# A fused attention, soft mixture and feed-forward kernel: the recurrence's transposes made whole, and the logits computed slot by slot

## The chip, the cores and the metric

One core of a Trainium2 chip runs the kernel. The metric is the device time of one execution in microseconds (us). Everything is float32, or float32 split into two rounded parts.

## What is computed

The input is r, k, v of shape (4 batches, 8 heads, 768 tokens, 48), a decay w and a bonus u per head. The reference runs three stages, one after the other:

```python
for t in range(S):                       # a linear-attention recurrence, per batch and head
    cur = einsum('bhd,bhe->bhde', u * k_t, v_t)
    y_t = einsum('bhd,bhde->bhe', r_t, state + cur)
    state = w * state + einsum('bhd,bhe->bhde', k_t, v_t)
x = y, as (3072 tokens, 384)
logits = x @ phi                         # soft mixture: 32 slots, 8 experts of 4 slots
disp = softmax(logits over tokens);  slot_in = disp.T @ x
slot_out = per expert: relu(slot_in @ w1) @ w2
x = softmax(logits over slots) @ slot_out
out = (relu(x @ w_in) ** 2) @ w_out      # feed-forward, 384 -> 2048 -> 384
```

## The kernel before

**Units.** The recurrence is cut into 6 chunks of 128 tokens and, inside a chunk, into 4 pairs of heads (hp = 0 to 3). A chunk and a pair make a unit, n = 4c + hp, 24 in all; a unit holds all 4 batches, and a chunk is worked in two halves of 64 tokens. The two heads of a pair lie at partitions 0 to 47 and 64 to 111 (HEAD_ROWS), so that TensorE's array is used as four 64x64 tiles: most products are 16 small matmuls, and the profile counts two MATMUL records for each (x32). In one unit TensorE does, in this order, own_step of the unit before (scores times values, L949), on hp = 1 only the logits of the chunk before (logit_parts, L880), scores_step (L911), keys_step (the next unit's keys transposed, turn_keys, L899), carried_step (queries times the old state, L934), state_step (keys times values, L922), carried_rest (L934), and turn_step (the output of the unit before transposed to tokens on partitions, turn_x, L890).

**Transposes and logits.** turn_keys and turn_x are ordinary matmuls against a piece of the identity, 16 of 64x64 or 48x48 each. logit_parts is 64 matmuls per chunk (x128 records) of 48 rows by 32 slots, the two heads of a pair kept apart in two halves of the PSUM tile turn_ps, which VectorE then adds (add_logits, L730). turn_ps has two banks and serves four uses in turn: the logits, the transposed keys, the transposed x, and the powers of the decay before the loop. So keys_step(n) waits for keep_x of the earlier unit (x_done), turn_step waits for keep_keys (k_done), and after the logits keys_step waits for VectorE's sum (lg_free).

**The other engines.** ScalarE does per unit keep_x (L532, two copies into x_sb), copy_y (L519, PSUM to x_t), keep_keys (L508) and scale_bonus (L501). VectorE does mask_scores (L701, L705), advance (L716, L720) and scale (L691). GpSimd does keep_state (L449) and turned_keys (L431), which weights the natural-order keys of a unit three ahead. SyncE issues the loads in a written order: per unit keys_in, two recept, values and one 512 KB piece of w1. Semaphores alone order the engines.

**Code.** The block of TensorE writes the chunk loop as a hardware loop, `with pe.Fori(0, CH) as c:` (L1033), whose body holds the four units of a chunk; all other engines have their 24 units written out. Later, groups 1 to 4 of the feed-forward stage are a hardware loop on TensorE, ScalarE and VectorE (L1220), with a body of 208 matmuls.

**Before the loop.** GpSimd makes the identity, masks (const_step), clears recept buffers, values of unit 3 and state_a (L424, the last of it after the load values_in[1]), makes fold4 (L438), then weights keys 0 to 2. VectorE computes powers of w; TensorE turns them (L1020) and VectorE copies them to kn_pow (L674). ScalarE clears PSUM and x_t (L538 to L544). Then keys_step and state_step of unit 0 run and the loop begins (L1033).

**After the loop.** own_step of unit 23, the logits of the last chunk (three pairs ahead of y_copied, the last pair behind it), turn_x into score_ps, the column maxima, gather (L1066, disp.T @ x), the experts (L1114, L1139), the mix, and the feed-forward stage (L1176, L1198), which runs from about 210 us to the end.

Of the kernel before, what the change touches and what calls it, by code (L numbers as in the profile page):

```python
# [12 lines left out]
P = 128  # L13
# [48 lines left out]
def program(nc, rk_t, rkv_n, w_t, u, phi, w1, w2, w_in, w_out, out):  # L62
# [35 lines left out]
    keys_n = [place(f"keys_n{i}", [P, B, 2, D]) for i in range(HP)]  # L98
# [5 lines left out]
    state_next = place("state_next", [P, HP, B, D])  # L104
# [3 lines left out]
    disp = place("disp", [P, TILES, SLOTS])  # L108
    x_t = place("x_t", [P, HP, B, P])
    q_pow = place("q_pow", [P, HP, SUB])  # L110
    state_b = place("state_b", [P, HP, B, D])
# [65 lines left out]
    with stack:  # L177
# [5 lines left out]
        with phase:  # L183
# [5 lines left out]
            turn_ps = bank("turn_ps", 2 * BANK)  # L189
# [18 lines left out]
        back_cleared = sem("back_cleared")  # L208
        ps_cleared = sem("ps_cleared")
# [25 lines left out]
        x_done = sem("x_done")  # L235
        logit_mm = sem("logit_mm")
# [62 lines left out]
        def _(sp):  # L299
# [4 lines left out]
            def load_params():  # L304
                by_head = u.rearrange("(a h d) -> h d a", h=2, d=D)
# [89 lines left out]
        def _(pool):  # L395
# [23 lines left out]
            pool.wait_ge(back_cleared, R_BUFS - 2)  # L419
            nc.gpsimd.memset(values[HP - 1][:, :, :], 0.0).then_inc(carried_done, 1)  # L420
            for hp in range(HP):
                if hp == HP - 1:
                    pool.wait_ge(values_in[1], 16)
                nc.gpsimd.memset(state_a[:, hp], 0.0).then_inc(state_a_ready, 1)  # L424

            def turned_keys(n):
# [4 lines left out]
                nc.gpsimd.tensor_tensor(keys_n[n % HP][:, :, :, :],  # L431
# [3 lines left out]

            for q in range(QUADS):
                rows = slice(SLOTS * q, SLOTS * (q + 1))
                chained(nc.gpsimd.tensor_copy(fold4[rows, :].rearrange("p (a s) -> p a s", s=SLOTS),  # L438
                                              ident[rows, rows].unsqueeze(1).broadcast_to([SLOTS, QUADS, SLOTS])))
# [15 lines left out]
            pool.wait_ge(kn_pow_done, 1)  # L455
            for n in range(HP - 1):
                turned_keys(n)
# [38 lines left out]
        def _(sc):  # L496
# [7 lines left out]
            def keep_keys(n):  # L504
# [3 lines left out]
                nc.scalar.activation(  # L508
                    keys[n % 2][0:PAIR].rearrange("p b (s t) -> p s b t", t=SUB),
                    turn_ps[0:PAIR, :].rearrange("p (s b t) -> p s b t", s=2, t=SUB)[:, :, 0:B], ACT.Copy,  # L510
                    scale=w_64_inv[0:PAIR, n % HP:n % HP + 1]).then_inc(k_done, 1)

            def copy_y(n):
# [4 lines left out]
                wait(sc, logit_mm, c + 1)  # L518
# [31 lines left out]
            for n in range(UNITS):  # L550
                if n >= 2:
                    keep_x(n - 2, turn_ps)
# [713 lines left out]
```

## Time and profile before

| | us |
|---|---|
| median of 3 runs | 448.79 |
| lowest, highest | 444.84, 472.27 |
| the profiled execution | 445.05 |
| its span, first to last instruction | 443.3 |

The profiled execution is one run, 3.74 us under the median; its span is 1.75 us shorter than its time. Times in rows are counted from the start of the span. Busy time of an engine says nothing by itself; what counts is which work or wait stands in the chain that ends last. PE is TensorE's matmuls, PEld its weight loads, DVE VectorE, ACT ScalarE, POOL GpSimd, SP SyncE, PEclk the clock granted to TensorE as a share of 2.4 GHz.

### The profile page before, as it was taken

The numbers are of one execution on the slowest core, as the hardware profiler recorded it, in microseconds if no ns is written. First come the engines' busy times: TensorE is split into PE (matmuls) and PEld (weight loads), VectorE is DVE, ScalarE is ACT, GpSimd is POOL, SyncE is SP. The second block draws the span as 40 slices with busy tenths as digits, with TensorE's granted clock in tenths as the row PEclk, the third lists the DMA queues.
The fourth block names the chain that finished last, engine by engine and source line by source line (L and its number), as shares of the span: only waits on it lengthen the run. The fifth ranks groups of instructions, "written<-read, shape, count | busy, mean of one in ns | idle before, by whom it ended". The sixth has DMA issues, their size and how long they took to land.

```text
span 443.3 us, 16892 instructions
## 1 busy us (share of the span) xinstructions
PE 390.5 (88%) x7284; PEld 354.4 (80%) x7284; DVE 245.6 (55%) x395; ACT 199.2 (45%) x351; POOL 56.0 (13%) x91
## 2 busy tenths in 40 slices
PE   0767799479699987996699999999999999999997
PEld 0666799478599842353699999999999999999996
DVE  6324387325366637115966655565665566566553
ACT  4214365323255511126345654565465455546542
POOL 4421124211232001105600000000000000000000
PEclk9968899866699968999699999999999999999999
DMA  5536478562469299995000020010010001001001
GB/s 142 166 104 206 151 243 242 174 204 88 138 227 310 63 368 371 375 404 185 1 0 1 1 72 1 1 71 0 0 70 1 0 0 71 0 0 71 0 1 71
DMA packets 29027, 50.93 MB, mean 115 GB/s; under 512 B 3777, under 2 KB 23233, under 8 KB 28609
## 3 DMA queue, kind: packets, MB, share of 16 engines
q1 hardware_dynamic: 28992, 50.44, 34.0%
q8 instruction: 26, 0.43, 0.4%
q14 instruction: 9, 0.07, 0.1%
HBM read 45.71 MB, written 4.72 MB: 114 GB/s over the span
## 4 chain that ended last, share of the span: by engine, by line
PE 86%; issue 7%; DVE 3%; SPq 1%; ACT 1%; DMA 1%; POOL 1%; DVEq 0%; POOLq 0%; ACTq 0%
PE out_ps L1198 46%; PE score_ps L911 7%; PE h_ps L1176 5%; PE turn_ps L890 4%; PE turn_ps L880 4%; PE turn_ps L899 3%; PE y_ps L934 3%; PE y_ps L949 3%; PE wide L1114 3%; PE inc_ps L922 3%; PE wide L1139 2%; PE wide L1066 1%; DVE act_lo L857 1%; ACT x_sb L532 1%; PE wide L1125 1%
## 5 line engine op out<-in xcount | busy, mean ns | idle before, releaser
L1198 PE MATMUL out_ps<-w_hi,act_hi 128*128 128x384 f32 x384 | 130.9, 341 | 5.1 <-DVE act_lo L857 5.1
L1198 PE MATMUL out_ps<-w_hi,act_lo 128*128 128x384 f32 x384 | 131.3, 342 | 0.0
L1198 PE MATMUL out_ps<-w_lo,act_hi 128*128 128x384 f32 x384 | 131.0, 341 | 0.0
L852 DVE TENSOR_TENSOR act<-relu_h 128x512 f32<-128x512 f32 x96 | 68.8, 716 | 78.7 <-ACT relu_h L620 78.7
L620 ACT ACTIVATE relu_h<-h_ps 128x512 f32<-128x512 f32 x96 | 57.3, 597 | 101.2 <-PE h_ps L1176 100.3
L1198 PEld LDWEIGHTS out_ps<-w_hi,act_hi 128*128 128x128 f32 x384 | 72.9, 190 | 6.2 <-ACT act_hi L623 3.8
L1198 PEld LDWEIGHTS out_ps<-w_lo,act_hi 128*128 128x128 f32 x384 | 73.2, 191 | 3.8
L1198 PEld LDWEIGHTS out_ps<-w_hi,act_lo 128*128 128x128 f32 x384 | 72.8, 190 | 0.0
L857 DVE TENSOR_TENSOR act_lo<-act,act_hi 128x512 fp32r<-128x512 f32 x96 | 68.4, 712 | 4.6 <-ACT act_hi L623 1.0
L623 ACT ACTIVATE act_hi<-relu_h 128x512 fp32r<-128x512 f32 x96 | 60.8, 634 | 3.9
L701 DVE TENSOR_TENSOR scores<-score_ps,ident_sub 128x512 f32<-128x512 f32 x24 | 16.6, 692 | 47.9 <-PE score_ps L911 47.9
L911 PE MATMUL score_ps<-queries,keys 48*64 48x128 f32 x768 | 35.0, 318 | 8.3 <-issue 8.3
L1176 PE MATMUL h_ps<-mix_t,gin 128*128 (+1 forms) x96 | 37.9, 396 | 0.4 <-DVE gin L834 0.4
L508 ACT ACTIVATE keys<-turn_ps,w_inv 112x512 f32<-112x512 f32 x24 | 16.5, 687 | 43.9 <-PE turn_ps L899 43.9
L911 PEld LDWEIGHTS score_ps<-queries,keys 48*64 48x64 f32 x768 | 28.0, 161 | 9.6 <-issue 9.6
L519 ACT ACTIVATE x_t<-y_ps 112x512 f32<-112x512 f32 x25 | 14.9, 597 | 29.5 <-PE turn_ps L880 20.2
L431 POOL TENSOR_TENSOR keys_n<-keys_in,kn_pow 128x384 f32<-128x384 f32 x24 | 24.6, 1028 | 28.2 <-DMA keys_in<-in_rkv_n 28.0
L899 PE MATMUL turn_ps<-ident_sub,keys_n 64*48 64x64 f32 x800 | 21.3, 247 | 7.3 <-POOL keys_n L431 7.3
L899 PEld LDWEIGHTS turn_ps<-ident_sub,keys_n 64*48 64x48 f32 x800 | 20.2, 146 | 7.5 <-issue 7.4
L949 PE MATMUL y_ps<-scores,values 64*48 64x64 f32 x800 | 19.3, 239 | 6.4 <-issue 6.1
L934 PE MATMUL y_ps<-queries,state_a 48*48 48x64 f32 x384 | 23.0, 233 | 0.0
L890 PE MATMUL turn_ps<-ident,x_t 48*64 48x48 f32 x768 | 19.1, 231 | 4.3 <-issue 4.2
(149 smaller groups left out, 436.9 us busy)
## 6 DMA issues: line engine op xcount, KB each, us to landing
w_sb<-in_w SPq DMA_DIRECT2D x21, 512.0 KB, 4.4
w_room<-in_w SPq DMA_DIRECT2D x4, 1536.0 KB, 13.5
keys_in<-in_rkv_n SPq DMA_DIRECT2D x24, 192.0 KB, 4.2
recept<-in_rk_t SPq DMA_DIRECT2D x48, 96.0 KB, 3.6
values<-in_rkv_n SPq DMA_DIRECT2D x24, 192.0 KB, 2.6
out_dram<-y_sb SPq DMA_DIRECT2D x5, 768.0 KB, 3.6
w_x<-in_w SPq DMA_DIRECT2D x2, 1536.0 KB, 13.4
w_w<-in_w SPq DMA_DIRECT2D x4, 768.0 KB, 10.0
```

The costliest lines, as they stand in the source:

```text
L431: nc.gpsimd.tensor_tensor(keys_n[n % HP][:, :, :, :], keys_in[n % K_BUFS][:, :, :].rearrange("p b (h d) -> p b h d", h=2), kn_pow[:, hp].u ...
L620: nc.scalar.activation(relu_h[f % 2][:, :], h_ps[f % 4][:, :], ACT.Relu).then_inc(relu_done, 1)
L623: nc.scalar.activation(act_hi[f % 4][:, :], relu_h[f % 2][:, :], ACT.Square).then_inc(act_hi_done, 1)
L852: nc.vector.tensor_tensor(act[f % 2][:, :], relu_h[f % 2][:, :], relu_h[f % 2][:, :], ALU.mult).then_inc(act_done, 1)
L857: nc.vector.tensor_tensor(act_lo[f % 4][:, :], act[f % 2][:, :], act_hi[f % 4][:, :].bitcast(F32), ALU.subtract).then_inc(act_lo_done, 1)
L890: last = nc.tensor.matmul(bank[HALVES[s], at:at + D], x_t[HEAD_ROWS[r], hp, b, HALVES[s]], ident[HEAD_ROWS[r], HEAD_ROWS[r]], start=True, ...
L899: last = nc.tensor.matmul(turn_ps[HEAD_ROWS[h], at:at + SUB], keys_n[i][HALVES[s], b, h], ident_sub[HALVES[s], :], start=True, stop=True)
L911: last = nc.tensor.matmul(score_ps[part, at:at + P], keys[hp % 2][rows, b, part], queries[hp][rows, b, s].rearrange("p k t -> p (k t)"), s ...
L934: return nc.tensor.matmul(y_ps[head_rows(b, h), at:at + SUB], state[HEAD_ROWS[h], hp, b], queries[hp][HEAD_ROWS[h], b, s, 0], start=(s == ...
L949: return nc.tensor.matmul(y_ps[head_rows(b, h), at:at + SUB], values[hp][HALVES[s], b, D * h:D * (h + 1)], scores[hp % 2][HALVES[s], h, b] ...
L1176: nc.tensor.matmul(h_ps[f % 4][:, :], gin[:, P * f:P * (f + 1)], mix_t[:, bass.ds(g * B, B), :], start=True, stop=True).then_inc(h_mm, 1)
L1198: last = nc.tensor.matmul(out_ps[t][:, 0:DM], a[f % 4][:, tok], w[:, f], start=(f == 0 and i == 0), stop=(f == NF - 1 and i == 2))
```

## The change

- turn_keys and turn_x become 4 whole transposes each (128x128, and 112 rows in). turn_ps is split into two banks: x_ps for x and the logits, kt_ps for the keys. For that keys_n gets 64 columns a head in place of 48, with the 16 extra cleared (GpSimd), and phi_sb is cleared before its load (VectorE; SyncE waits for it, phi_cleared).
- The logits are computed transposed: pair_logits is 8 matmuls, stationary phi (112x32), moving x_t (112x256), each pair in its own 32 columns of the array, so that each pair's 32 slots are rows of x_ps. ScalarE copies that to the new logits_t (keep_logits_t); token_logits, 4 matmuls with logits_t stationary and 32 columns of fold4 moving, adds the four pairs and turns the result to tokens; ScalarE copies it to logits (keep_logits). VectorE's add_logits goes.
- On hp = 1, keys_step moves ahead of the logits, keep_keys ahead of copy_y, and token_logits stands between state_step and carried_rest.
- Before the loop, TensorE gets two runs of 7 matmuls of the identity with itself (keep_awake), into score_ps. The powers are turned into x_ps and kt_ps, with no PSUM clear ahead of them; VectorE copies them in two. GpSimd weights the keys of unit 0 right after kn_pow, ahead of fold4 and of the last piece of state_a.
- After the loop, pair_logits of the last chunk stands whole behind y_copied.
- state_next and state_b change places in memory; state_b now lies on disp, which is written only after the loop.

```diff
-    keys_n = [place(f"keys_n{i}", [P, B, 2, D]) for i in range(HP)]
+    keys_n = [place(f"keys_n{i}", [P, B, 2, SECOND]) for i in range(HP)]
...
-            turn_ps = bank("turn_ps", 2 * BANK)
+            x_ps = bank("x_ps")
+            kt_ps = bank("kt_ps")
...
             pool.wait_ge(back_cleared, R_BUFS - 2)
+            for i in range(HP):
+                nc.gpsimd.memset(keys_n[i][:, :, :, D:], 0.0)
             nc.gpsimd.memset(values[HP - 1][:, :, :], 0.0).then_inc(carried_done, 1)
-            for hp in range(HP):
-                if hp == HP - 1:
-                    pool.wait_ge(values_in[1], 16)
+            for hp in range(HP - 1):
                 nc.gpsimd.memset(state_a[:, hp], 0.0).then_inc(state_a_ready, 1)
...
-            pool.wait_ge(kn_pow_done, 1)
-            for n in range(HP - 1):
+            pool.wait_ge(kn_pow_done, 2)
+            turned_keys(0)
+            pool.wait_ge(kn_done, 1)
+            for q in range(QUADS):
+                rows = slice(SLOTS * q, SLOTS * (q + 1))
+                chained(nc.gpsimd.tensor_copy(fold4[rows, :].rearrange("p (a s) -> p a s", s=SLOTS),
+                                              ident[rows, rows].unsqueeze(1).broadcast_to([SLOTS, QUADS, SLOTS])))
+            pool.wait_ge(values_in[1], 16)
+            nc.gpsimd.memset(state_a[:, HP - 1], 0.0).then_inc(state_a_ready, 1)
+            for n in range(1, HP - 1):
...
-                nc.scalar.activation(
-                    keys[n % 2][0:PAIR].rearrange("p b (s t) -> p s b t", t=SUB),
-                    turn_ps[0:PAIR, :].rearrange("p (s b t) -> p s b t", s=2, t=SUB)[:, :, 0:B], ACT.Copy,
-                    scale=w_64_inv[0:PAIR, n % HP:n % HP + 1]).then_inc(k_done, 1)
+                nc.scalar.activation(keys[n % 2][0:PAIR], kt_ps[0:PAIR, :].rearrange("p (b t) -> p b t", t=P), ACT.Copy,
+                                     scale=w_64_inv[0:PAIR, n % HP:n % HP + 1]).then_inc(k_done, 1)
...
-                wait(sc, logit_mm, c + 1)
+                wait(sc, lt_mm, c + 1)
...
-                tiles = x_sb[:, c * B:(c + 1) * B, 2 * D * hp:2 * D * (hp + 1)].rearrange("p (a i) (h d) -> p i h a d", i=2, h=2)
-                for i in range(2):
-                    spot = bass.AP(bank[:, :].tensor, bank[:, (BANK + D) * i:].offset,
-                                   [bank[:, :].ap[0], [BANK * (1 - 2 * i), 2], [2 * D, B // 2], [1, D]])
-                    last = nc.scalar.activation(tiles[:, i], spot, ACT.Copy)
+                for h in range(2):
+                    spot = bass.AP(bank[:, :].tensor, bank[:, SECOND * h:].offset,
+                                   [bank[:, :].ap[0], [2 * P, B // 2], [P + SECOND - 2 * SECOND * h, 2], [1, D]])
+                    at = 2 * D * hp + D * h
+                    last = nc.scalar.activation(
+                        x_sb[:, c * B:(c + 1) * B, at:at + D].rearrange("p (a i) d -> p a i d", i=2), spot, ACT.Copy)
                 last.then_inc(x_done, 1)
...
+            def keep_logits_t(c, bank):
+                sc.wait_ge(lt_mm, c + 2)
+                nc.scalar.activation(logits_t[:, :, :], bank[:, :].rearrange("p (b t) -> p b t", t=P),
+                                     ACT.Copy).then_inc(lt_done, 1)
+            def keep_logits(c, bank):
+                sc.wait_ge(logit_mm, c + 2)
+                nc.scalar.activation(logits[:, c * B:(c + 1) * B, :],
+                                     bank[:, 0:B * SLOTS].rearrange("p (b s) -> p b s", s=SLOTS),
+                                     ACT.Copy).then_inc(lg_free, 1)
...
             for n in range(UNITS):
+                c, hp = n // HP, n % HP
                 if n >= 2:
-                    keep_x(n - 2, turn_ps)
+                    keep_x(n - 2, x_ps)
+                if hp == 1 and n + 1 < UNITS:
+                    keep_keys(n + 1)
                 copy_y(n - 1)
+                if c > 0 and hp == 1:
+                    keep_logits_t(c - 1, x_ps)
                 if n + 1 < UNITS:
-                    keep_keys(n + 1)
+                    if hp != 1:
+                        keep_keys(n + 1)
                     scale_bonus(n + 1)
                 else:
                     sc.wait_ge(k_done, UNITS)
                     sc.sem_inc(k_done, 1)
-            keep_x(UNITS - 2, turn_ps)
+                if c > 0 and hp == 1:
+                    keep_logits(c - 1, x_ps)
+            keep_x(UNITS - 2, x_ps)
             copy_y(UNITS - 1)
+            keep_logits_t(CH - 1, kt_ps)
+            keep_logits(CH - 1, kt_ps)
...
+            nc.vector.memset(phi_sb[:, :, :, :], 0.0).then_inc(phi_cleared, 1)
...
-            TILES_64 = tuple(itertools.product(range(2), range(2)))
-            def logit_parts(pairs):
-                for hp in pairs:
-                    for b in range(B):
-                        for r, s in TILES_64:
-                            at = BANK * r + SLOTS * b
-                            last = nc.tensor.matmul(turn_ps[HALVES[s], at:at + SLOTS], x_t[HEAD_ROWS[r], hp, b, HALVES[s]],
-                                                    phi_sb[HEAD_ROWS[r], b % 2, hp], start=(hp == 0 and b == 0), stop=True,
-                                                    skip_group_check=True)
-                return last
+            def pair_logits(bank):
+                pairs = x_t[0:PAIR].rearrange("p h (a i) t -> p h i a t", i=2)
+                spots = bank[:, :].rearrange("p (a i t) -> p i a t", i=2, t=P)
+                for turn in range(2):
+                    for hp in range(HP):
+                        last = nc.tensor.matmul(spots[SLOTS * hp:SLOTS * (hp + 1), turn], phi_sb[0:PAIR, turn, hp],
+                                                pairs[:, hp, turn], start=True, stop=True)
+                last.then_inc(lt_mm, 1)
+            def token_logits(bank):
+                for b in range(B):
+                    last = nc.tensor.matmul(bank[:, SLOTS * b:SLOTS * (b + 1)], logits_t[:, b], fold4[:, 0:SLOTS],
+                                            start=True, stop=True)
+                last.then_inc(logit_mm, 1)
             def turn_x(hp, bank):
                 for b in range(B):
-                    for r, s in TILES_64:
-                        at = BANK * r + D * b
-                        last = nc.tensor.matmul(bank[HALVES[s], at:at + D], x_t[HEAD_ROWS[r], hp, b, HALVES[s]],
-                                                ident[HEAD_ROWS[r], HEAD_ROWS[r]], start=True, stop=True)
+                    last = nc.tensor.transpose(bank[:, P * b:P * b + PAIR], x_t[0:PAIR, hp, b], ident[0:PAIR, 0:PAIR])
                 last.then_inc(x_mm, 1)
             def turn_keys(i):
                 for b in range(B):
-                    for s, h in TILES_64:
-                        at = BANK * s + SUB * b
-                        last = nc.tensor.matmul(turn_ps[HEAD_ROWS[h], at:at + SUB], keys_n[i][HALVES[s], b, h],
-                                                ident_sub[HALVES[s], :], start=True, stop=True)
+                    last = nc.tensor.transpose(kt_ps[:, P * b:P * (b + 1)],
+                                               keys_n[i][:, b].rearrange("p h d -> p (h d)"), ident[:, :])
                 last.then_inc(kt_mm, 1)
...
-                pe.wait_ge(x_done, n)
+                pe.wait_ge(k_done, n)
...
-                pe.wait_ge(k_done, n + 3)
+                pe.wait_ge(x_done, n + 2)
                 settled()
-                turn_x(hp, turn_ps)
+                turn_x(hp, x_ps)
...
+            def keep_awake(count, bank):
+                for i in range(count):
+                    nc.tensor.matmul(bank[:, 0:P], ident[:, :], ident[:, :], start=True, stop=True)
             pe.wait_ge(const_step, IDENT)
+            keep_awake(7, score_ps)
             pe.wait_ge(pow_t_done, 1)
-            pe.wait_ge(ps_cleared, 1)
             for hp in range(HP):
-                for r, s in TILES_64:
-                    at = BANK * r + D * hp
-                    last = nc.tensor.matmul(turn_ps[HALVES[s], at:at + D], kn_powt[HEAD_ROWS[r], hp],
-                                            ident[HEAD_ROWS[r], HEAD_ROWS[r]], start=True, stop=True)
+                for r, bank in enumerate((x_ps, kt_ps)):
+                    for part in HALVES:
+                        last = nc.tensor.matmul(bank[part, D * hp:D * (hp + 1)], kn_powt[HEAD_ROWS[r], hp],
+                                                ident[HEAD_ROWS[r], HEAD_ROWS[r]], start=True, stop=True)
             last.then_inc(pow_n_done, 1)
+            keep_awake(7, score_ps)
             pe.wait_ge(const_step, MASKS)
             pe.wait_ge(kn_done, 1)
             turn_keys(0)
-            pe.wait_ge(ps_cleared, 2)
+            pe.wait_ge(ps_cleared, 1)
             pe.wait_ge(values_in[0], 16)
             unit_state(0)
-            pe.wait_ge(ps_cleared, 4)
+            pe.wait_ge(ps_cleared, 3)
+            pe.wait_ge(lt_done, 1)
             pe.wait_ge(params_in, 4 * 16)
+            pe.wait_ge(const_step, FOLD)
             with pe.Fori(0, CH) as c:
                 for hp in range(HP):
                     n = c * HP + hp
                     own_step(n - 1, (hp - 1) % HP)
                     if hp == 1:
+                        keys_step(n + 1, (hp + 1) % HP)
                         pe.wait_ge(x_done, n + 1)
                         settled()
-                        logit_parts(range(HP)).then_inc(logit_mm, 1)
+                        pair_logits(x_ps)
                     scores_step(n, hp)
+                    if hp != 1:
+                        keys_step(n + 1, (hp + 1) % HP)
+                    carried_step(n, hp)
+                    state_step(n + 1, (hp + 1) % HP)
+                    if hp == 1:
+                        pe.wait_ge(lt_done, c + 1)
+                        settled()
+                        token_logits(x_ps)
+                    carried_rest(n, hp)
                     if hp == 1:
                         pe.wait_ge(lg_free, c + 1)
-                    keys_step(n + 1, (hp + 1) % HP)
-                    carried_step(n, hp)
-                    state_step(n + 1, (hp + 1) % HP)
-                    carried_rest(n, hp)
                     turn_step(n - 1, (hp - 1) % HP)
             pe.wait_ge(pmax_done, 1)
             nc.tensor.transpose(wide[1][0:SLOTS, 0:P], slot_t[:, 1, :], ident[:, :]).then_inc(pmax_t_done, 1)
             own_step(UNITS - 1, HP - 1)
-            pe.wait_ge(x_done, UNITS + 1)
-            logit_parts(range(HP - 1))
             pe.wait_ge(y_copied, UNITS + 1)
-            logit_parts((HP - 1,)).then_inc(logit_mm, 1)
+            pair_logits(kt_ps)
             turn_x(HP - 1, score_ps)
             pe.wait_ge(dmax_done, 1)
             nc.tensor.matmul(wide[1][:, P:P + SLOTS], ones[:, :], slot_t[0:SLOTS, 0, :], start=True, stop=True
                              ).then_inc(bmax_done, 1)
+            pe.wait_ge(lt_done, CH + 1)
+            token_logits(kt_ps)
```

## Rows read from the trace of the kernel before

**Rows 1.** The page: the clock granted to PE, 40 slices of 11.1 us
```profile
PEclk9968899866699968999699999999999999999999
```

**Rows 2.** Windows, one for each chunk (columns as in the first line)
```profile
core 0: us, PE busy (x) PEld busy (x) DVE busy (x) ACT busy (x) POOL busy (x), PEclk, DMA share, GB/s
15.20:47.00 31.80, 22.26 (x907) 20.94 (x900) 13.70 (x22) 9.60 (x19) 6.50 (x10) 0.84 0.48 152
47.00:64.70 17.70, 17.29 (x896) 16.60 (x896) 11.18 (x20) 9.57 (x20) 4.33 (x7) 0.91 0.64 209
64.70:80.80 16.10, 15.75 (x896) 15.12 (x896) 11.76 (x22) 9.62 (x20) 4.44 (x6) 1.00 0.90 276
80.80:119.20 38.40, 25.01 (x910) 23.69 (x911) 14.58 (x23) 9.71 (x20) 7.75 (x11) 0.68 0.45 141
119.20:136.50 17.30, 16.93 (x896) 16.26 (x889) 10.62 (x20) 9.62 (x21) 4.85 (x7) 0.92 0.67 218
136.50:153.00 16.50, 16.16 (x924) 15.50 (x928) 10.86 (x17) 8.84 (x20) 1.54 (x2) 1.00 0.53 181
```

**Rows 3.** The chain in chunk 0 (start, us, what)
```profile
21.47 2.48 issue
...
26.35 1.93 issue
...
38.96 2.22 issue
...
43.72 2.58 issue
```

**Rows 4.** The chain in chunk 3
```profile
80.83 6.07 issue
...
88.00 1.71 PE score_ps L911 x32
```

**Rows 5.** DMA of chunk 0, then of chunk 3: packets, MB, share
```profile
q8 instruction: 7, 0.11, 1.5%
...
q8 instruction: 9, 0.15, 1.9%
```

**Rows 6.** The chain in a warm unit of chunk 1
```profile
57.91 0.45 PE y_ps L949 x32
58.35 0.90 PE score_ps L911 x32
59.26 0.45 PE turn_ps L899 x32
...
61.28 0.45 PE y_ps L949 x32
```

**Rows 7.** Timeline of PE: whole transposes between 128x4 matmuls
```profile
179.75 0.60 PE L1114 MATMUL wide<-w_sb,slot_t 128*4 128x512 f32 x3
...
180.28 1.09 PE L1098 MATMUL wide<-ident,hid 128*128 128x128 f32 x8
181.30 0.60 PE L1114 MATMUL wide<-w_sb,slot_t 128*4 128x512 f32 x3
```

**Rows 8.** Chain and timeline: forms near those of the new logits
```profile
199.46 2.76 PE wide L1160 x24
...
168.65 0.85 PE L1090 MATMUL wide<-fold,slot_in 128*128 128x32 f32 x6 [2.00 <-DVE slot_in L784]
```

**Rows 9.** Timeline before the loop
```profile
7.60 0.44 SPq L310 DMA_DIRECT2D phi_sb<-in_phi  x1
...
10.76 0.26 POOL L424 MEMSET state_a<- 128x192 f32 x1 [4.36 <-DMA values<-in_rkv_n]
...
12.50 2.90 POOL L431 TENSOR_TENSOR keys_n<-keys_in,kn_pow 128x384 f32<-128x384 f32 x3
```

**Rows 10.** Groups by line, DVE: busy and mean ns | idle before
```profile
L705 DVE COPY_PREDICATED scores<-mask_sub,score_ps 128x512 f32<-128x512 uint32 x24 | 17.7, 739 | 0.8
L701 DVE TENSOR_TENSOR scores<-score_ps,ident_sub 128x512 f32<-128x512 f32 x24 | 16.6, 692 | 47.9 <-PE score_ps L911 47.9
```

More of the change, by code:

```diff
@@ L3 @@
 from contextlib import ExitStack
-import itertools
 F32 = mybir.dt.float32
@@ L108, in program @@
     disp = place("disp", [P, TILES, SLOTS])
+    state_b = place("state_b", [P, HP, B, D], at=loads_end)
+    assert place.end <= cursor[0]
     x_t = place("x_t", [P, HP, B, P])
     q_pow = place("q_pow", [P, HP, SUB])
-    state_b = place("state_b", [P, HP, B, D])
+    logits_t = place("logits_t", [P, B, P])
+    state_next = place("state_next", [P, HP, B, D])
     phi_sb = place("phi_sb", [P, 2, HP, SLOTS])
@@ L235, in program @@
         x_done = sem("x_done")
+        lt_mm = sem("lt_mm")
+        lt_done = sem("lt_done")
         logit_mm = sem("logit_mm")
@@ L430, in turned_keys @@
                 wait(pool, inc_done, n - HP + 1)
-                nc.gpsimd.tensor_tensor(keys_n[n % HP][:, :, :, :],
+                nc.gpsimd.tensor_tensor(keys_n[n % HP][:, :, :, 0:D],
                                         keys_in[n % K_BUFS][:, :, :].rearrange("p b (h d) -> p b h d", h=2),
@@ L434, in turned_keys @@
                                         ALU.mult).then_inc(kn_done, 1)
[L436 to L439, printed above, removed]
             def keep_state(n):
@@ L673, in _ @@
             ve.wait_ge(pow_n_done, 1)
-            nc.vector.tensor_copy(
-                kn_pow[:, :, :, :].rearrange("p a h d -> p h a d"),
-                turn_ps[:, :].rearrange("p (r q) -> p r q", r=2)[:, :, 0:HP * D].rearrange("p r (a d) -> p r a d", d=D)
-                ).then_inc(kn_pow_done, 1)
+            for half, bank in enumerate((x_ps, kt_ps)):
+                nc.vector.tensor_copy(kn_pow[:, :, half], bank[:, 0:HP * D].rearrange("p (a d) -> p a d", d=D)
+                                      ).then_inc(kn_pow_done, 1)
             chained(nc.vector.tensor_tensor(q_pow[0:PAIR], q_pow[0:PAIR],
@@ L724, in advance @@
                     ve.sem_inc(state_next_done, 1)
-            def add_logits(c):
-                ve.wait_ge(logit_mm, c + 2)
-                halves = turn_ps[:, :].rearrange("p (r q) -> p q r", r=2)[:, 0:B * SLOTS]
-                nc.vector.reduce_sum(logits[:, c * B:(c + 1) * B, :].rearrange("p b s -> p (b s)"), halves, AX.X
-                                     ).then_inc(lg_free, 1)
             scale(0)
@@ L739, in _ @@
                 c, hp = n // HP, n % HP
-                if c > 0 and hp == 1:
-                    add_logits(c - 1)
                 mask_scores(n)
@@ L921, in unit_state @@
                             at = BANK * s + D * b
-                            last = nc.tensor.matmul(inc_ps[rows, at:at + D], keys_n[hp][part, b, h],
+                            last = nc.tensor.matmul(inc_ps[rows, at:at + D], keys_n[hp][part, b, h, 0:D],
                                                     values[hp][part, b, D * h:D * (h + 1)], start=True, stop=True)
```

9 lines of the change are left out of this document (4 added, 5 removed).

## The prediction

> **What bounds the kernel now.** I read the page first, then windows cut at the chunks, then the chain of waits inside a slow and a fast chunk, then the DMA queues of the same stretches, and last the timeline before the loop. The page's clock line is the first hint: it falls to 0.6 in two places, some 70 us apart, both inside the recurrence [rows 1]. Windows by chunk give the shape: the same 896 matmul records take 31.8 us in chunk 0 and 38.4 us in chunk 3, but 17.7, 16.1, 17.3 and 16.5 us in the other four [rows 2]. In the fast chunks PE is busy for 98% of the time and every step follows the last: a warm unit repeats after 61.28 - 57.91 = 3.37 us [rows 6], so three plain units take 10.1 us of chunk 2's 16.1 and the one with the logits 6.0. In the slow chunks the chain has gaps named "issue", in which PE waits for nothing that the profile shows: four of 1.9 to 2.6 us, 9.2 us in sum, in chunk 0 [rows 3], and one of 6.07 us at the very start of chunk 3, where the hardware loop jumps back for the third time [rows 4]. The DMA view names the cause that I take: the instruction queue moved 7 packets in chunk 0 and 9 in chunk 3 [rows 5], 0.11 and 0.15 MB; the other four chunks have none. TensorE's loop body is fetched once, kept for two rounds, then fetched again whole. 896 records in 7 pieces is 128 matmuls with their weight loads for a piece. The returns from the idle rows are at 23.95, 28.28, 41.18 and 46.30 [rows 3]; the seven pieces make five steps from the first of these to the last, 22.35 / 5 = 4.5 us for a piece, against 16.1 / 7 = 2.3 us in which a warm PE consumes one [rows 2]. A fetching chunk runs at the fetch's pace, and the gaps also cost clock (0.84 and 0.68 granted [rows 2]: in part 1.2 GHz in place of 2.4). Scores take 1.71 us there against 0.90 warm [rows 4, 6].
>
> **The change, part by part.** The profiled execution took 445.05 us with a span of 443.3, so 1.75 us lies around the span, and it is 3.74 us under the median of 448.79. All sums are made on the span.
>
> Records of a chunk. Keys and x go from 32 records a unit each to 4 each (a transpose is one record, rows 7: eight in one group of eight), the logits from 128 to 16 + 8. What stays is 4 x 128. New body: 4 x (128 + 8) + 24 = 568 in place of 896, that is 568 / 128 = 4.4 pieces in place of 7.
>
> Before the loop. Now the keys of unit 0 are weighted at 12.50 [rows 9], because POOL first waits for values_in[1] (memset at 10.76) and makes fold4. The new order needs only kn_pow, which is ready near 7.5 (the old copy took 0.56 us and the new two about as much together), plus 1 us for the weighting (2.90 / 3). Then come the transposes (0.5 to 1 us), keep_keys and scale_bonus (0.7 us each), so that scores can start at about 11.4 in place of 16.3. The last phi load is issued at 7.60 [rows 9] and is the other gate, near 10.1; fold4 is ready there too. POOL gets four small memsets and SyncE a wait for one small memset, all hidden unless the phi load slips. Keys 1 still wait for values_in[1] and end near 12, before PE asks. I take the loop's start at 10.4 in place of 15.2; bounds are 9.5 and 13 (the 14 identity matmuls late, or a load late). The identity matmuls run where PE idles, so they cost nothing, and may leave the clock up.
>
> Chunk 0. The first idle row stands in unit 1, 23.95 - 15.2 = 8.8 us after the loop's start [rows 3], at a fixed place in the code; the same count of records reaches into unit 1 of the new body. 10.4 + 8.8 = 19.2, then two more pieces at 4.5 make 28.2, and about 70 remaining records 2.1: chunk 0 ends at 30.3 in place of 47.0. That is 16.7 us less so far, 4.8 from the start and 11.9 from the chunk. Bounds: 27 (pieces come in 3.5) and 34 (PE cold, near twice as slow [rows 4, 6]).
>
> A warm chunk. Eight whole transposes between tiled matmuls take 181.30 - 180.28 = 1.02 us, and the first starts 0.09 later than the 0.43 us pitch of the matmuls before it would have it [rows 7]. I read that as 0.115 us for a transpose and 0.1 for each change of the array's tiling. So keys cost 4 x 0.115 + 2 x 0.1 = 0.66 in place of 0.45 [rows 6], and x, now as many records as the keys, the same: fewer records, but a unit of 3.37 + 0.42 = 3.79 us, not a shorter one. The logits: 24 records of 512 columns took 2.76 us, four in parallel [rows 8], so 16 of 256 take 0.92; token_logits is 8 records at (0.85 - 0.28) / 5 = 0.114 (0.28 is the last one's own time, 1.09 - 7 x 0.115 [rows 7]), 0.92; with tiling changes the logits unit is 3.79 + 1.12 + 1.12 = 6.0, as before. Its waits have cover: the early keys step hides keep_x (the 0.3 us wait goes), scores and state_step (some 1.7 us) hide copy_y and keep_logits_t (1.2 us), and behind PE's wait for lg_free only turn_step is queued. ScalarE gets two more copies a chunk, about 0.9 us beside 9.6 busy of 16.1 [rows 2]. Chunk: 3 x 3.79 + 6.0 = 17.4 us in place of 16.1. Bounds of a unit: 3.15, below which the loop of scores, two mask steps (0.69 and 0.74 [rows 10]) and own_step does not let it go even if PE gets shorter, and 4.5 (a tiling change at 0.28, a whole matmul latency). I take 3.79, the row of the same operation.
>
> The Trainium skill, "TensorEngine Tiling (Array Packing)", section "Key Properties", says that a change of tiling mode drains the engine. Here the row shows 0.09 to 0.1 us for it, and with no drain at all the sum would be 0.4 us a unit smaller, 8 us over the loop.
>
> Chunks 1 to 5. The body no longer fills what held 7 to 9 pieces, so I expect no second fetch; the feed-forward loop, of 208 records a round, is not refetched either. Chunk 3 then costs as the others: 5 x 17.4 = 87.0, and 1.0 for a cold start of one of them (chunks 1 and 4 now take 17.7 and 17.3 against 16.3). DMA then carries chunk 2's load, share 0.90 at 276 GB/s [rows 2], for five chunks in a row; at 17.4 us a chunk this is less dense than that, so it holds. The loop ends at 30.3 + 88.0 = 118.3 in place of 153.0: -34.7 us.
>
> After the loop. All four pairs' logits now stand behind y_copied (0.92), then turn_x and, on ScalarE, three copies before the first Exp; against the old 1.3 us of logits with a 1.1 us gap inside, I count 0, between -1 and +2.6 (one fetch gap [rows 3]). The rest is moved whole.
>
> Sum: 443.3 - 34.7 = 408.6, plus 1.75 around it = 410.35, say 410. The median before is 3.7 above the profiled execution, which I leave to the range.
>
> **The rivals.**
> (a) The second fetch stays. The loop was kept for two rounds and lost at the third, which a body of fixed size and a full store do not explain by themselves. Then chunk 3 costs 6.1 + 4.4 x 4.5 + about 5 of cold work = 31 in place of 17.4: 424 us. For it: the loss came after two clean rounds. Against: the shorter later loop has no such gap. The Trainium skill, "Runtime: NRT & Kernel Launch", section "Instruction fetch mechanics", says that a taken branch out of the window held forces a fetch; the trace agrees for chunk 3 but not for the jumps into chunks 1 and 2.
> (b) Tiling changes cost a latency each: 0.18 more, four a unit, 24 units: +17, 427 us.
> (c) They cost nothing and VectorE's mask chain bounds: 3.15 a unit and 5.4 with logits, 14.9 a chunk, five times 2.5 less: 398 us.
> (d) The other side: the clock stays at 1.2 GHz in the loop, as fewer, longer weight-bound transposes replace dense small matmuls. PE's steps then cost 1.9 times as much (1.71 / 0.90 [rows 4, 6]), a chunk some 31 us, 13.6 more: all five, 478 us. It decides from three cold chunks on (34.7 / 13.6 = 2.6): 451 us there. For it: the clock did fall in the slow chunks; against: it fell after gaps of 2 us and more, and these go. The Trainium skill, "TensorE: Matmul & The Clock Gate", section "Part 4: PE-mode transpose", says that transposes do not count as busy the same way; no stretch of this trace is made of them alone.
>
> **How the numbers follow.** Forecast 0.60, (a) 0.18, (b) 0.07, (c) 0.09, (d) 0.06. The forecast's own range is 402 to 418. The range of 8 in 10 takes in (c) and (a) and reaches 397 to 434. About 2% (9 us) is what a measurement of this kernel tells from no change. All cases but (d) are faster by more than that; part of (d) with two or three cold chunks is near no change: faster 0.88, same 0.06, slower 0.06.
>
> **What would show it.** Right: instruction packets only in chunk 0 (four or five), no gap at the start of chunk 3, windows of 16.5 to 18 us for chunks 1 to 5 at a clock of 0.95 or more, first scores at 11 to 12 us, L911 still 0.90. Wrong: a gap of 3 us or more at any later jump back; a warm unit under 3.3 or over 4.1; PEclk 0.6 across a chunk without a gap; POOL's keys_n late for keys_step, with a wait on keys_in before it in PE's chain.

## The result and the profile after

The changed kernel takes 414.3 us (median of 4 runs, 413.24 to 415.19) against 446.81 us before (median of 4, 443.8 to 472.27): a ratio of 0.929, 95% interval 0.922 to 0.937. The ratio is taken over the executions in the fast state, so the one of 472.27 us is not in it. The forecast was 410, range 397 to 434. The profiled execution has a span of 412.4 us, 30.9 less than before.

The page of the changed kernel: busy time, clock, instruction queue and chain.

```profile
PE 389.8 (95%) x5184; PEld 338.2 (82%) x5184; DVE 243.3 (59%) x391; ACT 204.6 (50%) x363; POOL 58.7 (14%) x95
...
PEclk9896999999999899988999999999999999999999
...
q8 instruction: 14, 0.23, 0.3%
...
PE 88%; DVE 4%; DMA 3%; issue 2%; SPq 1%; ACT 1%; DVEq 0%; ACTq 0%
```

Three things are to be read here. PE is busy for 389.8 us against 390.5, with 2100 records fewer. The clock's two hollows of [rows 1] have shrunk to one slice at 6. And 14 packets are left of 26 on q8, the instruction queue that this document counts. (A second one, q14, moved 8 packets against 9; four of them fell between 36.4 and 122.6 us, where PE has no gap.) Most of the time came out of the idle time of PE: 22.6 us are left of 52.8. But the two busy sums are not the same work: 6.7 us of the new one are the identity matmuls ahead of the loop, and chunk 3 alone lost 8.1 us of busy time (25.01 to 16.91), in which PE had worked at the lower clock.

Windows of the changed kernel, one for each stretch (what stands before the loop, six chunks, what follows), to be laid beside [rows 2]:

```profile
0.00:11.50 11.50, 9.34 (x96) 8.52 (x97) 8.43 (x33) 5.88 (x7) 8.99 (x31) 1.00 0.54 142
11.50:36.40 24.90, 20.90 (x572) 16.32 (x576) 13.04 (x22) 9.28 (x17) 7.71 (x11) 0.84 0.65 208
36.40:54.40 18.00, 17.91 (x572) 14.89 (x572) 11.49 (x20) 10.56 (x22) 5.21 (x8) 0.94 0.64 218
54.40:71.50 17.10, 17.01 (x574) 14.00 (x577) 11.33 (x21) 10.55 (x22) 5.61 (x8) 1.00 0.79 261
71.50:88.50 17.00, 16.91 (x572) 13.89 (x576) 11.17 (x21) 10.56 (x22) 6.55 (x10) 1.00 0.80 259
88.50:105.50 17.00, 16.91 (x572) 13.89 (x573) 11.54 (x21) 10.55 (x22) 6.29 (x9) 1.00 0.79 258
105.50:122.60 17.10, 17.01 (x571) 13.94 (x571) 10.09 (x15) 9.27 (x21) 1.54 (x2) 1.00 0.50 172
```

Chunk 3 fell from 38.4 to 17.0 us; it has no gap at its start, and no packet of q8 moved from 36.4 to 122.6. Chunk 0 fell from 31.8 to 24.9. The loop starts at 11.5 in place of 15.2. The three together are 32.0 us. Chunk 4 gained 0.3, while chunks 1, 2 and 5 lost 0.3, 1.0 and 0.6 us: a warm chunk is longer than the unhindered ones of before. From the loop's end to the end of the span it is 289.8 us (412.4 - 122.6) against 290.3.

The chain in one warm unit of the changed kernel (start, us, what), beside [rows 6]; the two lines of the old unit that [rows 6] leaves out stand behind it:

```profile
67.82 0.59 PE y_ps L968 x32
68.41 0.88 PE score_ps L930 x32
69.29 0.59 PE kt_ps L918 x4
69.88 0.37 PE y_ps L953 x16
70.25 0.46 PE inc_ps L941 x30
70.71 0.23 PE y_ps L953 x16
70.94 0.53 PE x_ps L912 x4
71.47 0.59 PE y_ps L968 x32
```

```profile
59.71 0.23 PE y_ps L934 x16
...
60.63 0.65 PE turn_ps L890 x32
```

A plain unit takes 71.47 - 67.82 = 3.65 us against 3.37. The keys account for all of it: their four transposes take 0.59 against 0.45 for 32 records, and the step behind them, which changes the tiling back, 0.37 against 0.23, together 0.28 more. Those of x take less than before, 0.53 against 0.65, and the own_step behind them more, 0.59 against 0.45: 0.02 in sum.

And the chain in chunk 0, where the time is still being lost:

```profile
14.84 1.39 issue
...
18.56 1.86 PE x_ps L898 x16
20.43 1.55 PE score_ps L930 x32
...
29.48 2.54 issue
...
36.37 1.04 PE y_ps L968 x32
37.40 1.49 PE score_ps L930 x32
```

Two gaps named issue are left, 3.9 us, and after each the granted clock is down, at 0.51 from 18.0 to 21.5 us and at 0.50 from 31.7 to 38.5: scores take 1.5 us in place of 0.88, pair_logits 1.86 in place of 1.00.

### The profile page after: what moved, and what is told of

Read it like the earlier page. It is cut to its first block, busy times and chain, and to the rows that moved or that the text cites. A ratio compares the mean times of both kernels' runs of the same rounds, so it can differ in the third digit from the quotient of the medians.

```text
span 412.4 us, 12711 instructions
## 1 busy us (share of the span) xinstructions
PE 389.8 (95%) x5184; PEld 338.2 (82%) x5184; DVE 243.3 (59%) x391; ACT 204.6 (50%) x363; POOL 58.7 (14%) x95
## 4 chain that ended last, share of the span: by engine, by line
PE 88%; DVE 4%; DMA 3%; issue 2%; SPq 1%; ACT 1%; DVEq 0%; ACTq 0%
PE out_ps L1231 49%; PE score_ps L930 6%; PE h_ps L1209 5%; PE kt_ps L918 4%; PE y_ps L953 4%; PE y_ps L968 4%; PE x_ps L912 3%; DMA w_w<-in_w 3%; PE inc_ps L941 3%; PE wide L1147 2%; PE x_ps L898 2%; PE x_ps L905 1%; SPq L379 1%; PE score_ps L1036 1%; DVE act_lo L877 1%
## 5 line engine op out<-in xcount | busy, mean ns | idle before, releaser
L517 ACT ACTIVATE keys<-kt_ps,w_inv 112x512 f32<-112x512 f32 x24 | 16.5, 687 | 28.9 <-PE kt_ps L918 28.9
L930 PE MATMUL score_ps<-queries,keys 48*64 48x128 f32 x768 | 27.4, 281 | 2.6 <-issue 2.5
L930 PEld LDWEIGHTS score_ps<-queries,keys 48*64 48x64 f32 x768 | 22.3, 140 | 5.7 <-issue 5.7
L953 PE MATMUL y_ps<-queries,state_b 48*48 48x64 f32 x384 | 21.3, 226 | 1.4 <-issue 1.4
L953 PE MATMUL y_ps<-queries,state_a 48*48 48x64 f32 x384 | 20.4, 225 | 0.0
L721 DVE TENSOR_TENSOR queries<-recept,q_pow 112x512 f32<-112x512 f32 x24 | 20.4, 848 | 0.0
L539 ACT ACTIVATE x_sb<-x_ps 128x192 f32<-128x192 f32 x46 | 12.7, 330 | 14.7 <-PE x_ps L912 14.7
L1209 PEld LDWEIGHTS h_ps<-mix_t,gin 128*128 128x128 f32 x96 | 18.2, 190 | 0.9 <-ACT gin L631 0.8
L953 PEld LDWEIGHTS y_ps<-queries,state_a 48*48 48x48 f32 x384 | 14.1, 122 | 5.0 <-issue 4.7
## 6 DMA issues: line engine op xcount, KB each, us to landing
w_room<-in_w SPq DMA_DIRECT2D x4, 1536.0 KB, 13.5
```

Of the source, the lines that this page charges most:

```text
L517: nc.scalar.activation(keys[n % 2][0:PAIR], kt_ps[0:PAIR, :].rearrange("p (b t) -> p b t", t=P), ACT.Copy, scale=w_64_inv[0:PAIR, n % HP:n ...
L721: nc.vector.tensor_tensor(queries[n % Q_BUFS][0:PAIR].rearrange("p b s k t -> p (b s) k t")[:, :, 0], recept[n % R_BUFS][0:PAIR].rearrange ...
L930: last = nc.tensor.matmul(score_ps[part, at:at + P], keys[hp % 2][rows, b, part], queries[hp][rows, b, s].rearrange("p k t -> p (k t)"), s ...
L953: return nc.tensor.matmul(y_ps[head_rows(b, h), at:at + SUB], state[HEAD_ROWS[h], hp, b], queries[hp][HEAD_ROWS[h], b, s, 0], start=(s == ...
L1209: nc.tensor.matmul(h_ps[f % 4][:, :], gin[:, P * f:P * (f + 1)], mix_t[:, bass.ds(g * B, B), :], start=True, stop=True).then_inc(h_mm, 1)
```

## The experiments

Two theories stood against each other. **Length:** the loop body of 896 records was just too long to be kept by TensorE's instruction store, and the change gained by making it shorter, whatever it put in place. **Work:** the change gained by its parts, larger transposes and fewer matmuls, or by keeping the clock up. E1, E2, E3, E8 and E9 are one execution each; the differences read from them are some 20 us and more.

**E1, the kernel before with fewer records.** In the loop, the logits of one pair of heads only are computed; the other three are left out of the in-loop logits.

```diff
-                        logit_parts(range(HP)).then_inc(logit_mm, 1)
+                        logit_parts(range(1)).then_inc(logit_mm, 1)
```

> The kernel before, with the logits inside the loop taken from one of the four pairs only: a loop body of 800 matmul records in place of 896 (three quarters of the in-loop logits are left out). Theory, the body's length decides: if 800 records fit, chunk 3 has no idle row of 6 us at its start, no instruction packets, and lasts 15 us in place of 38.4; the time falls by more than 25 us, though only 1.6 us of matmuls a chunk (9 us in all) is taken out. Rival, the second fetch comes from something else at that point (the third jump back as such, the loads beside it): chunk 3 still shows the gap and 8 or 9 packets and the time falls by 9 to 13 us only.

409.64 us, beside 462.67 for the kernel before on the same chip; against the median of 446.8 it is 37 us less, for 96 records taken out of each chunk. Part of that is the work left out: a warm chunk is 1.4 us shorter than the 16.1 of [rows 2], some 8 us over six chunks. Chunks 2 to 5 last 14.7 us each, chunk 0 27.8. This is the kernel with the old transposes and the old logits, without one line of the change.

**E2 and E3, the changed kernel with a longer body.** The products of state_step are issued three and four times over, with the same result.

```diff
             def state_step(n, hp):
...
                 settled()
+                for _ in range(2):       # E2; range(3) in E3
+                    state_products(hp)
                 unit_state(hp)
```

> The changed kernel with the products of state_step issued three times over (same operands, same result): a loop body of 568 + 2 x 128 = 824 records. Theory of length: 824 lies beside the 800 of the other run, so both show a second fetch or neither. If neither: chunks 1 to 5 last 17.0 + 8 x 0.46 = 20.7 us each, chunk 0 some 5 to 8 us more than before the padding, time 414 + 24 = 438 to 442. If there is a second fetch: another 20 us, 460. Rival, the change cured it in some other way than by length: no second fetch here, whatever the body holds.

> The same with the state products issued four times: 568 + 3 x 128 = 952 records, more than the 896 of the kernel before. Theory of length: instruction packets again in a chunk after chunk 0, in one or more of the jumps back, with a gap of about 6 us and a chunk paced at 4.5 us for each 128 records (over 35 us); time above 470. Rival (cured in another way): chunks 1 to 5 at 17.0 + 12 x 0.46 = 22.5 us, time 414 + 33 + 8 for chunk 0 = 455, and packets in chunk 0 alone.

E2: 433.84 us, chunks 1 to 5 at 20.0 us, no second fetch. E3: 535.1 us, 101 us more for 128 records in each chunk. The instruction queue on E3's page:

```profile
q8 instruction: 62, 1.02, 0.8%
```

Two windows of its loop:

```profile
115.00:155.00 40.00, 31.77 (x1066) 26.53 (x1059) 14.94 (x22) 12.03 (x25) 5.20 (x8) 0.79 0.40 133
155.00:195.00 40.00, 27.90 (x867) 23.65 (x868) 11.82 (x19) 9.26 (x20) 5.23 (x8) 0.76 0.32 104
```

62 packets against 14 (53 of them in the loop, some 9 a round), and 40 us hold about one round. The gains of the change are gone, all of them and more, with its parts all in place. That settles length against work, for chunk 3.

**E8, the kernel before again, and E9, with 864 records.** E9 leaves one pair of four out of the in-loop logits (`range(3)`).

> The kernel before, unchanged, for a second trace of it: its times spread from 441 to 472 us. Theory, a body of 896 records is just over what is held, and how many rounds after the first fetch again decides the time, some 20 us each: a time near 445 goes with 7 packets in chunk 0 and 8 or 9 in one later chunk, one near 465 with two such chunks. Rival, the spread has another cause (clock, loads): the packets are the same 26 in all, whatever the time.

> The kernel before with the in-loop logits taken from three of the four pairs (a quarter of the in-loop logits is left out): 864 records, between the 824 that were kept and the 896 that were not. Theory of length: either kept (17 or so packets in all, time 411 to 415 us) or fetched again in one or two rounds (440 or more); nothing between. Rival, the loss grows gradually with length: a time near 425.

E8: 444.94 us, and the same picture as in the first trace: 7 packets in chunk 0, 9 in chunk 3, 26 in all, and this gap where [rows 4] has 6.07:

```profile
80.54 7.11 issue
```

The runs near 465 us were not caught in a trace, so what makes them is open. E9: 414.66 us, 17 packets, seven of them for the loop (the last at 44.3 us, just inside chunk 1, and none from there to the loop's end), and these windows of chunks 0, 1 and 3:

```profile
15.70:43.80 28.10, 19.79 (x866) 18.55 (x861) 12.59 (x22) 9.38 (x19) 5.31 (x8) 0.88 0.52 159
43.80:59.50 15.70, 15.35 (x864) 14.68 (x865) 11.15 (x21) 9.59 (x20) 5.16 (x8) 1.00 0.82 259
75.20:90.90 15.70, 15.35 (x866) 14.66 (x868) 12.94 (x22) 9.61 (x20) 6.74 (x9) 1.00 0.95 289
```

Thirty-two records fewer than the kernel before, and 30 us less. The edge lies between 864 and 896 in this code, whose place in memory was not varied, and it is sharp: kept for all six rounds on one side; on the other (896) lost once, twice in the same place; at 952 lost in every round. The Trainium skill, "Runtime: NRT & Kernel Launch", section "Instruction fetch mechanics", gives TensorE's store as 2048 instructions in pieces of 16 KiB. A record here is two instructions, so the edge seen is, as an estimate from the record counts, between 1728 and 1792 plus waits and branches, some way under that figure; the piece size agrees (0.11 MB in 7 packets).

**E4, E5, the identity matmuls.** E4 leaves out both runs of keep_awake, E5 the second.

```diff
             last.then_inc(pow_n_done, 1)
-            keep_awake(7, score_ps)
```

> The changed kernel without the two runs of 7 identity matmuls before the loop. Theory: the second run is on the path (PE is busy with it from 6.5 to 9.8 us while the keys of unit 0 are ready at 8.9), so the loop starts 0.5 to 1 us earlier, but the clock is down when it starts and unit 0 and 1 cost up to 2 us more: 413 to 416 us against 414.3, no difference that can be told. Rival, the identity matmuls carry much of the gain by keeping the clock up in chunk 0: 418 us or more. Other rival, they only delay: 412 or less.

> The changed kernel with the first run of 7 identity matmuls kept and the second left out. Theory: start of the loop 0.6 us earlier as in the run without both; whether the clock is up there decides between 413 and 416 us. If the second run is what raises the clock before 11.5 us, this one behaves as the run without both.

E4 413.98 us (410.87 to 415.53, ratio to before 0.936, interval 0.924 to 0.949), E5 411.25 (410.32 to 414.26, ratio 0.928, 0.917 to 0.940). Neither can be told from the changed kernel's 414.3. The loop starts no earlier without the second run: E5 at 11.55. My expectation was wrong there, for fold4 holds it, as the chain of E5 shows (E4 starts at 11.51 with the same wait):

```profile
7.79 1.11 POOL keys_n L437
...
10.77 0.30 POOL fold L461
11.08 0.47 issue
11.55 1.11 PE y_ps L968 x32
```

The identity matmuls do change PE's pace at the start of the loop (own_step at 11.5 takes 0.67 us with both, 1.11 with the first only, 1.10 with none; the granted clock reads 1.00 there in all three), and yet the median is no worse without them. In the traces chunk 0 was even shorter: 21.9 us in E4 and 22.1 in E5, at a granted clock of 1.00 and 0.99, against 24.9 at 0.84. That fits a chunk 0 paced by its instruction packets; whether the identity matmuls or chance lowered the clock later in chunk 0 of the changed kernel, one trace of each cannot tell.

**E6, the other parts without the whole transposes.** Built on the kernel before: its turn_keys, turn_x and turn_ps, with the new logits and the new order before the loop; the logits lie in the two banks of inc_ps, no identity matmuls. In the loop on hp = 1:

```diff
-                        pe.wait_ge(x_done, n + 1)
+                        pe.wait_ge(state_b_done, n + 1)
+                        pe.wait_ge(state_next_done, n + 1)
                         settled()
-                        logit_parts(range(HP)).then_inc(logit_mm, 1)
+                        pair_logits(inc_ps[:, 0:BANK])
...
+                        token_logits(inc_ps[:, BANK:2 * BANK])
+                        carried_rest(n, hp)
+                        turn_step(n - 1, (hp - 1) % HP)
+                        pe.wait_ge(lg_free, c + 1)
+                        state_step(n + 1, (hp + 1) % HP)
```

> Keys and x transposed by 16 small matmuls each as in the kernel before (turn_ps of two banks, no identity matmuls), with the new logits (in the two banks of inc_ps, state_step behind them on hp = 1) and the new order before the loop: a body of 768 + 24 = 792 records. Theory, length alone brings the gain and the whole transposes cost 0.28 us a unit: no second fetch, plain units at 3.37 us, the logits unit at 5.5, a chunk 15.6 in place of 17.0, chunk 0 one or two us longer for its extra piece or two; 406 to 409 us, faster than the changed kernel. Rival, whole transposes are part of the gain: 414 us or more. Rival, 792 records don't fit: over 425.

414.66 us (413.41 to 416.24; ratio 0.936, 0.922 to 0.949): the same as the changed kernel, where I expected 406 to 409. A warm chunk did come down, to 15.8 us, with plain units at 3.37:

```profile
83.69 0.46 PE y_ps L975 x32
84.15 0.90 PE score_ps L937 x32
85.06 0.45 PE turn_ps L925 x32
...
87.08 0.45 PE y_ps L975 x32
```

What it won there, some 5 us over chunks 1 to 5, it lost in chunk 0, which took 29.4 us (11.43 to 40.85) against 24.9: 792 records need 7 packets, the last at 41.0 us, where 568 need 5. So the whole transposes are worth what they cost: 0.28 us more in each warm unit, and in the fetching round 4.5 us less than in E6 (7.5 less by the trace of E4, which has no identity matmuls either). E6 is not an exact pair to either kernel, as its logits lie in another place and state_step stands behind them, but the two medians cannot be told apart.

**E7, the keys product back behind scores on hp = 1.**

> The changed kernel with the keys product of hp = 1 back behind scores_step (and keep_keys behind keep_logits_t). Theory: pair_logits waits some 0.3 us for keep_x, and token_logits finds its copy a little later or earlier by as much; a logits unit 0.2 to 0.5 us longer, 415 to 417 us. Rival: no difference, 414.

414.35 us (413.01 to 415.42). A chunk is 17.26 us in place of 17.03 in the trace, which is the 0.2 us expected for each logits unit; over six chunks, 1.4 us cannot be told in the time. The early keys product is worth that and no more.

**E10, E11, E12, fewer tiling changes.** All three keep only the first identity run. E10 puts turn_x right behind turn_keys on hp = 0, 2 and 3, E11 puts both behind carried_rest, and E12 moves the wait for fold4 to its first use as well.

```diff
 # E11, in the loop of TensorE
-                    if hp != 1:
-                        keys_step(n + 1, (hp + 1) % HP)
                     carried_step(n, hp)
...
                         pe.wait_ge(lg_free, c + 1)
+                    else:
+                        keys_step(n + 1, (hp + 1) % HP)
                     turn_step(n - 1, (hp - 1) % HP)
```

> The changed kernel with the second run of identity matmuls left out, and, on hp = 0, 2 and 3, turn_x moved right behind turn_keys, so that the array changes its tiling twice in a unit and not four times. Theory, a change of tiling costs 0.05 to 0.1 us: plain units 3.65 - 0.1 to 0.2 us, three a chunk, 18 in all: 2 to 3.5 us less than the 411.3 of the run with the first identity matmuls only, 408 to 409 us. Rival, tiling changes cost nothing and the transposes are bound by their weight loads: 411, units at 3.65. Other rival, turn_x now waits for copy_y: units longer, over 412.

> First identity run only, and on hp = 0, 2 and 3 turn_keys moved behind carried_rest, right ahead of turn_x; ScalarE then does scale_bonus ahead of keep_keys there. In the run with turns together right behind scores, turn_x no longer lay between the carried products and own_step, and own_step stood waiting for them. Theory, that cover was what was lost, and two tiling changes a unit are worth 0.15 to 0.2 us: plain units at 3.45 to 3.5 in place of 3.65, chunks of 16.5, 408 us. Rival, keys now come too late: scores_step waits for keep_keys (0.2 + 0.69 us behind the keys against 0.98 us of cover), units of 3.65 or more, 411 us or more.

> The same, and TensorE's wait for fold4 moved from ahead of the loop to the first use, ahead of token_logits. Theory: fold4, ready at 11.0 us, holds the loop's start at 11.5; without it the loop starts at about 10.8 (unit_state and own_step), scores at about 12 as scale_bonus is ready only then: 0 to 0.7 us less than the run beside it. Rival: the start moves but chunk 0, paced by its instruction packets, ends no earlier: no difference.

E10: 418.45 us (416.76 to 423.62), longer than E5, the kernel that it was built on. Its chain shows both effects:

```profile
54.54 0.38 PE x_ps L912 x4
...
55.76 0.28 PE y_ps L953 x15
56.04 0.16 issue
56.20 0.81 PE y_ps L968 x29
```

The transposes of x fell from 0.53 to 0.38, one change of tiling saved; but own_step now stands directly behind the carried products that it waits for, with a gap and a longer step, and the units went to 3.7 to 3.9. That is 0.35 us for a warm chunk; the larger part of E10's loss stands in chunk 0, 26.5 us at a granted clock of 0.76 against E5's 22.1 at 0.99, and what makes it is open. E11, in which ScalarE also does scale_bonus ahead of keep_keys: 411.65 us (411.16 to 412.24), two of three plain units at 3.58, the third at 3.67, and chunks at 16.88 in place of 17.03. So the cover was what E10's units had lost; the gain is 0.05 us a unit, less than the 0.15 to 0.2 that I gave, and the time cannot be told from E5's 411.25. E12: 411.12 us (410.04 to 412.96; ratio to before 0.925, interval 0.916 to 0.935): the loop starts at 10.94 in place of 11.54 and ends at 118.1 in place of 119.15; the times of E11 and E12 overlap. Its four times all lie below the four of the changed kernel, but they were not taken side by side and the intervals of the two ratios overlap: 3 us better is likely, not shown.

## Why the prediction came out right, step by step

**What bounds the kernel** was read rightly, and E1, E3, E8 and E9 show the part that was only argued: the second fetch follows the number of records in the body, with the change's other parts and without them. What the forecast left as rival (a), that the second fetch stays, was ruled out by the first trace, and E9 shows how near it was in the kernel before: a quarter of the logits' records would have been enough.

**Before the loop** was off by 1.1 us: 11.5 in place of 10.4. Two steps failed, and they tie. One is "fold4 is ready there too": its four copies took 2.10 us where the trace of before had 1.33, and ended at 11.06. The other is that the identity matmuls cost nothing. The keys of unit 0 are ready at 8.9, but the second run ends at 9.84, and the chain of the changed kernel goes through it:

```profile
6.56 3.28 PE score_ps L1036 x14
9.84 0.85 PE kt_ps L918 x4
10.70 0.75 PE inc_ps L941 x32
```

Taking out the run alone gained nothing (E5, 11.55), as fold4 still holds the loop; with the wait for fold4 moved too, it starts at 10.94 (E12). The forecast also had the keys weighted from 7.5 us on; they were from 7.79.

**Chunk 0** is the term that was mis-sized: 24.9 us in place of 19.9. It holds two gaps of 3.9 us in sum and 20.9 us of PE work that takes 16.9 when warm. The 4 us between these are slow steps: the clock was at 1.2 GHz for 8 of the chunk's 24.9 us, 0.84 over the chunk, as in [rows 2]. I had priced that only as the upper bound of 34 us for the chunk's end; it ended at 36.4, outside it. The clock is not all of it. Traces of the same 568 records at a granted clock of 0.99 to 1.00 show 21.9 (E4), 22.1 (E5) and 22.7 us (E12), still 2 to 3 us over the forecast. The pace of the pieces fits as the other part: the five packets started at 13.5, 17.9, 23.2, 29.3 and 35.1 us, 5.4 us apart (5.0 in E4), where 4.5 was taken over from before; no run varies it by itself. The forecast's first gap, near unit 1, came in unit 0 (14.84).

**A warm chunk** was forecast at 17.4 and is 17.0. A unit has 3.65 us against 3.79, near, but by two errors that partly cancel. The keys cost 0.28 us more than before, where 0.21 was forecast. x costs 0.02 more, where 0.21 was forecast too: the forecast took the old price of x to be that of the keys, 0.45, and the old trace has 0.65 for it. The logits unit, 58.10 to 64.17, is 6.07 us against 6.0. Five of them, with the cold start of chunk 1, make 86.2 in place of 88.0.

**After the loop** 0 was forecast, and it is -0.5.

Sum: 408.6 + 1.1 + 5.0 - 1.8 - 0.5 = 412.4, the measured span.

Of the rivals, (b) and (c) bracketed the unit (3.15 and 4.5) and neither came: the steps behind the transposes (0.14 us longer) and E10 (0.15 less for x behind the keys) show that a tiling change is not free, though E11, with two fewer in a unit, won only 0.05 us. (d), the clock staying down, did not come: 1.00 in chunks 2 to 5, with eight whole transposes in each unit. The Trainium skill, "TensorE: Matmul & The Clock Gate", section "Part 4: PE-mode transpose", which says that transposes do not count as busy in the same way, is not contradicted, as 128 records in each unit of 136 are ordinary matmuls; here it had no price.

The stage behind the loop gained only 0.5 us, although the granted clock in its first 14.6 us was 1.00 against 0.77. Its chain in the changed kernel:

```profile
144.68 1.75 SPq L379
146.47 2.07 SPq L379
148.58 12.13 DMA w_w<-in_w
160.75 2.76 PE wide L1172 x32
```

The last experts' w2 is issued only when the first hidden products are done, and lands behind the other loads (12 us from issue to landing); TensorE stands 0.93 us for it, between 159.8 and 160.75. The trace of before shows PE in that place, [rows 7], with nearly the same sum. Moving these loads was not tried.

## What to carry to other kernels

Count the instructions in the body of a hardware loop on TensorE as one counts memory: past an edge, here between 864 and 896 matmul records, each with its weight load, a round costs what its fetch costs: here 4.2 (E9) to 5.6 us (the changed kernel) for each 128 records of chunk 0, the lower clock included. The sign is idle time named issue at the same places of the code, packets on the instruction queue in that stretch and no other; look for it before counting matmuls, and test it by leaving a few records out. When the body fits, the first round still pays for every record, so a form with fewer and longer instructions can win back there what it costs when warm (E6: equal times).

## What the runs showed that I had not expected

That a body can be half kept: 896 records are fetched once, held for two more rounds and lost in the fourth, at the same place in both traces (80.8 and 80.5 us). Why the fourth is open. That the cost of the edge is so steep: 32 records are worth 30 us in one direction (E9), 128 beyond 824 cost 101 us in the other (E3), of which about 10 are their own work by the step from the changed kernel to E2 (19.5 us for 256). And that TensorE's own products are a wait: own_step directly behind the carried products stands 0.14 to 0.16 us and then takes 0.66 us or more in place of 0.59 (E10); with the transposes laid between them the gap is gone (E11). The profile calls the gap issue; that it is own_step's wait for carried_done is read from the code and from this pair of runs.
